# Rotary attention and a gated MLP: the first batch's loads and rotations moved between engines

## What is computed

```python
def rotate(x):
    x1, x2 = (x[..., :half], x[..., half:])
    return np.concatenate([x1 * cos - x2 * sin, x1 * sin + x2 * cos], axis=-1)
q_rot, k_rot = (rotate(q), rotate(k))
scores = scale * np.matmul(q_rot, k_rot.transpose(0, 1, 3, 2))
scores = scores - np.max(scores, axis=-1, keepdims=True)
attn = np.exp(scores)
attn = attn / (np.sum(attn, axis=-1, keepdims=True) + 1e-09)
x = np.matmul(attn, v)                    # heads side by side: (4, 576, 512)
h = np.maximum(x @ w_in, 0.0)             # (4, 576, 1024)
conv_out = sum over k of conv_w[k] * h shifted by k - 1 positions
y = (h * 1.0 / (1.0 + np.exp(-conv_out))) @ w_out
```

## Time and profile before

| | us |
|---|---|
| median of 3 runs | 656.71 |
| profiled execution | 655.78 |
| its span, first to last instruction | 653.7 |
| TensorE busy (matmul) | 515.2 (79%) |
| VectorE busy | 511.8 (78%) |
| ScalarE busy | 406.1 (62%) |
| GpSimd busy | 295.1 (45%) |
| mean granted TensorE clock | 0.957 of full |

### The profile page before, as it was taken

The page is one execution under the profiler, slowest core; times in us unless marked ns, Lnnn a source line. Parts: engine busy times, 40 slices in busy tenths (PEclk is TensorE's granted clock), DMA queues, the critical chain, the costliest instruction groups (busy, mean ns, idle before and its releaser), DMA issues.

```text
span 653.7 us, 11977 instructions
## 1 busy us (share of the span) xinstructions
PE 515.2 (79%) x3552; PEld 471.4 (72%) x3552; DVE 511.8 (78%) x882; ACT 406.1 (62%) x907; POOL 295.1 (45%) x329
## 2 busy tenths in 40 slices
PE   0068888889587888869687988888959888887987
PEld 0058776789586777769586867778958777777976
DVE  6978878579988888659997888848998788865652
ACT  1247988755556877745456787855555587875552
POOL 4414777734551456414451456523544145640221
PEclk9999999989799999999979999997979799999989
DMA  5976000314452000223454000041345200000011
GB/s 185 245 194 261 1 1 2 125 64 127 129 154 64 2 2 2 80 78 99 128 164 117 2 2 2 2 153 51 118 127 159 59 1 2 1 2 2 1 37 37
DMA packets 22773, 48.72 MB, mean 75 GB/s; under 512 B 3120, under 2 KB 7344, under 8 KB 21936
## 3 DMA queue, kind: packets, MB, share of 16 engines
q1 hardware_dynamic: 22704, 47.87, 24.1%
HBM read 28.98 MB, written 4.72 MB: 52 GB/s over the span
## 4 chain that ended last, share of the span: by engine, by line
PE 28%; DVE 28%; issue 18%; ACT 16%; DMA 5%; POOL 2%; SPq 1%; ACTq 1%; DVEq 0%; POOLq 0%
DVE conv L715 9%; PE banks L355 8%; DVE u L724 5%; PE banks L383 4%; ACT conv L553 3%; DVE PT_lo L702 3%; PE banks L386 3%; ACT P_first L499 3%; DVE Q L646 3%; PE banks L327 2%; ACT PT_hi L518 2%; PE banks L328 2%; ACT hid L545 2%; DVE neg_max L669 1%; DMA Q<-K 1%
## 5 line engine op out<-in xcount | busy, mean ns | idle before, releaser
L669 DVE TENSOR_REDUCE neg_max<-banks 128x1 f32<-128x576 f32 x144 | 108.5, 756 | 39.9 <-PE banks L328 34.1
L518 ACT ACTIVATE PT_hi<-banks 128x512 fp32r<-128x512 f32 (+1 forms) x160 | 95.1, 597 | 67.6 <-PE banks L355 63.3
L715 DVE SCALAR_TENSOR_TENSOR conv<-hid,taps,conv 128x288 f32<-128x288 f32 x128 | 97.3, 760 | 36.1 <-ACT conv L553 32.0
L327 PE MATMUL banks<-K,Q 128*128 128x288 f32 x256 | 86.3, 351 | 43.0 <-DMA K<-K 31.7
L867 POOL TENSOR_TENSOR u_lo<-u,u_hi 128x288 fp32r<-128x288 f32 x64 | 53.9, 844 | 133.2 <-ACT u_hi L564 133.2
L417 PE MATMUL banks<-u_hi,wo_hi 128*128 128x288 f32 x256 | 80.6, 315 | 40.8 <-ACT y_sb L570 25.6
L851 POOL TENSOR_SCALAR P_first<-P_first,recip 128x576 f32<-128x576 f32 x68 | 50.2, 747 | 126.5 <-DVE recip L686 126.5
L702 DVE TENSOR_TENSOR PT_lo<-banks,PT_hi 128x512 fp32r<-128x512 f32 x128 | 86.9, 684 | 25.0 <-ACT PT_hi L518 23.7
L355 PE MATMUL banks<-ident,P_first 128*128 128x128 f32 (+1 forms) x400 | 78.1, 292 | 27.6 <-DVE PT_lo L702 17.8
L383 PE MATMUL banks<-PT_hi,V 128*128 128x288 f32 x320 | 90.9, 314 | 1.4 <-DVE PT_hi L706 1.3
L327 PEld LDWEIGHTS banks<-K,Q 128*128 128x128 f32 x256 | 50.9, 199 | 52.6 <-issue 32.1
(11 more groups left out here) (75 smaller groups left out, 1304.0 us busy)
## 6 DMA issues: line engine op xcount, KB each, us to landing
xc<-qk_dram SPq DMA_DIRECT2D x28, 288.0 KB, 2.8
xs<-qk_swapped_dram SPq DMA_DIRECT2D x28, 288.0 KB, 3.8
v_raw<-v_rows_dram SPq DMA_DIRECT2D x4, 1280.0 KB, 5.4
KL<-Q SPq DMA_DIRECT2D x32, 144.0 KB, 3.6
Q<-K SPq DMA_DIRECT2D x32, 144.0 KB, 3.6
K<-K SPq DMA_DIRECT2D x32, 144.0 KB, 2.7
y_dram<-y_sb SPq DMA_DIRECT2D x8, 576.0 KB, 3.4
wi_raw<-w_in_dram SPq DMA_DIRECT2D x1, 2048.0 KB, 7.8
```

Source lines behind the costliest of these rows:

```text
L327: nc.tensor.matmul(out, Q[:, h, qc], K[:, h, cols], start=True, stop=False)
L518: nc.scalar.activation(PT_hi[0:m, kt, 0:FULL * 128], bank[0:m, :], ACT.Copy)\
L669: nc.vector.tensor_reduce(out=neg_max[:, c:c + 1], in_=banks[:, 2 * (t % 2):2 * (t % 2) + 2, 0:HALF], axis=AX.XY, op=ALU.max, negate=True) ...
L715: nc.vector.scalar_tensor_tensor(out=conv[:, n % 2, :], in0=hid[:, slot, first:first + HALF], scalar=taps[:, f, k:k + 1], in1=conv[:, n % ...
```

## The change

Only the first batch's preparation is touched:

- ScalarE issues the loads of all eight heads (`load_first`), SyncE the tables, the moves, and what comes behind them. SyncE's moves now go by pairs (`prepare_first`): both heads' KL, then both q, then both k.
- ScalarE loads the table of the exponential (`load_table`) ahead of its first high part.
- The product by sines is VectorE's (`rotate_first`), no longer GpSimd's.
- VectorE does heads 0 to 3 first, then the first two maxima; the rotations of heads 4 to 7 lie between the further first tiles (`first_maxima` with `between`). ScalarE's high parts and exponentials are ordered to fit.

```diff
+            def prepare_first():
+                for pair in range(PAIRS):
+                    two = (2 * pair, 2 * pair + 1)
+                    for j in two:
+                        sp.wait_ge(rope_lo, j + 1)
+                        move_kl(0, j)
+                    for j in two:
+                        move_q(0, j)
+                    for j in two:
+                        move_k(0, j)
+                    if pair == 0:
                         sp.dma_start(ident[:, :], ident_in).then_inc(consts_in, 16)
                         sp.dma_start(taps[:, :, :], conv_w).then_inc(consts_in, 16)
+                    if pair == 1:
                         sp.dma_start(v_raw[:, :, :, :], v_rows[0, :, :, :, :]).then_inc(v_in, 16)
...
-            prepare(0, starting=True)
+            prepare_first()
             load_weights(wi_raw, w_in, wi_in)
             load_weights(wo_raw, w_out, wo_in)
...
+            def load_first(j):
+
+                c, w = rope_buffers(j, True)
+                loaded = (qk_more_in if j % 4 >= 2 else qk_in)[j % 2]
+                if j >= 4:
+                    act.wait_ge(rope_lo, j - 3)
+                act.dma_start(c, qk[0, j, :, :]).then_inc(loaded, 16)
+                act.dma_start(w, qk_swapped[0, j, :, :]).then_inc(loaded, 16)
+
+            for j in range(4):
+                load_first(j)
             act.wait_ge(tables_in, N_TABLES)
-            for j in range(H):
-                rope_high(0, j, starting=True)
-            for tile in FIRST_TILES[:-1]:
-                exp_tile(0, *tile)
+            load_table(ACT.Exp)
...
             act.wait_ge(consts_in, N_CONSTS)
             act.wait_ge(rope_lo, H)
             attention(0, True)
...
-            def first_maxima(b):
+            def first_maxima(b, between=()):
+                rest = iter(between)
                 max_tile(b, 0, 0)
                 max_tile(b, 0, 1)
+                for j in itertools.islice(rest, 1):
+                    rope_first(j)
                 max_tile(b, 0, 2)
...
+            def rotate_first(j):
+                _, w = rope_buffers(j, True)
+                times_cos(0, j, starting=True)
+                nc.vector.tensor_tensor(w, w, sin_t[:, :], ALU.mult).then_inc(sin_done, 1)
+                rope_add(0, j, starting=True)
+
+            def rope_first(j):
+                rotate_first(j)
+                rope_low(0, j, starting=True)
...
-            first_maxima(0)
+            first_maxima(0, range(4, H))
...
             nc.gpsimd.memset(QT[:, :, :].bitcast(F32), 0.0).then_inc(zeroed, 1)
-            pool.wait_ge(tables_in, N_TABLES)
-            for j in range(H):
-                times_sin(0, j, starting=True)
```

More of the change, by code:

```diff
@@ L1 @@
+import itertools
 import concourse.bass as bass
@@ L230, in _, with load_qk @@
         def _(sp):
[L231 to L236, removed]
+            def load_qk(b, j):
+                c, w = rope_buffers(j, False)
+                sp.dma_start(c, qk[b, j, :, :]).then_inc(qk_in[j % 2], 16)
+                sp.dma_start(w, qk_swapped[b, j, :, :]).then_inc(qk_in[j % 2], 16)
             def move_kl(g, j):
@@ L257, in store_y, with prepare @@
                 sp.dma_start(y_out[b, :, :, half * HALF:(half + 1) * HALF], y_sb[:, :, :]).then_inc(y_stored, 16)
[L259 to L262, removed]
+            def prepare(b):
+                for j in range(2):
+                    load_qk(b, j)
                 for j in range(1, H + 3):
@@ L265, in prepare @@
                         sp.wait_ge(rope_lo, b * H + j)
[L266 to L271, removed]
+                        if j + 1 < H:
+                            load_qk(b, j + 1)
+                        move_kl(b, j - 1)
                     if 2 <= j <= H + 1:
@@ L275, in prepare @@
                         move_k(b, j - 3)
-                    if not starting and j == 6:
+                    if j == 6:
                         store_y(b - 1, 0)
-                    if starting and j == 5:
+            def prepare_first():
[9 more added lines that the diff above has]
+                    if pair == 0:
                         sp.dma_start(ident[:, :], ident_in).then_inc(consts_in, 16)
                         sp.dma_start(taps[:, :, :], conv_w).then_inc(consts_in, 16)
-                    if starting and j == 6:
+                    if pair == 1:
                         sp.dma_start(v_raw[:, :, :, :], v_rows[0, :, :, :, :]).then_inc(v_in, 16)
@@ L620, in weights_high @@
                 nc.scalar.activation(hi, raw, ACT.Copy).then_inc(w_hi_done, 1)
-            act.wait_ge(tables_in, N_TABLES)
-            for j in range(H):
-                rope_high(0, j, starting=True)
-            for tile in FIRST_TILES[:-1]:
-                exp_tile(0, *tile)
+            def load_first(j):
[7 more added lines that the diff above has]
+                load_first(j)
+            act.wait_ge(tables_in, N_TABLES)
+            load_table(ACT.Exp)
+            rope_high(0, 0, starting=True)
+            rope_high(0, 1, starting=True)
+            load_first(4)
+            load_first(5)
+            rope_high(0, 2, starting=True)
+            load_first(6)
+            rope_high(0, 3, starting=True)
+            load_first(7)
+            exp_tile(0, *FIRST_TILES[0])
+            exp_tile(0, *FIRST_TILES[1])
+            rope_high(0, 4, starting=True)
+            exp_tile(0, *FIRST_TILES[2])
+            exp_tile(0, *FIRST_TILES[3])
+            rope_high(0, 5, starting=True)
+            exp_tile(0, *FIRST_TILES[4])
+            rope_high(0, 6, starting=True)
+            rope_high(0, 7, starting=True)
             act.wait_ge(consts_in, N_CONSTS)
@@ L796, in first_maxima @@
                 reciprocals(b, 0, 2)
+                for j in rest:
+                    rope_first(j)
                 normalise_group(b, 2)
+            def rotate_first(j):
[6 more added lines that the diff above has]
+                rope_low(0, j, starting=True)
             def normalise_group(b, k):
```

16 lines of the change are left out of this document (8 added, 8 removed).

## The result

| | before | after |
|---|---|---|
| median of the comparison's runs, us | 656.75 (4 runs) | 669.79 (4 runs) |
| ratio | 1 | 1.0202, 95% interval 1.0156 to 1.0248 |
| profiled execution, span | 655.78, 653.7 | 670.29, 668.5 |
| mean granted TensorE clock | 0.957 | 0.937 |

The forecast was 660.5 (657.0 to 664.0). The sign was right, the time is outside the range. Neither of the two signs by which the prediction would have been wrong in kind came: the idle time ahead of the weights' copy is there, and what follows is later.

A forecast was written before the change was run, and what follows sets the result against it. It took VectorE's chain and the weights' landing as the late points, the later setting what follows: chain 0.2 later, weights +4.3 us. Added to 655.78 or 656.71, this gives 660.1 or 661.0; forecast 660.5 us, range 657.0 to 664.0.

The forecast's parts named there:

- two signs by which the prediction would have been wrong in kind: Idle time before the first weights' copy under 3 us, or present but later stages less than 3 us later.
- Start of VectorE: First product on head 0: put at 6.9 against 7.04, as the loads' own queue gains almost nothing.
- Rotations: All on VectorE: 3.75 us per head alone, heads 2 and 3 ending at 20.3, table load hidden.
- So I take 3.1 each.: Three chained moves on SyncE from 12.8, between 2.4 and 4.94 each: TensorE starts at 22.2 instead of 31.7.
- the meeting with GpSimd: GpSimd's four instructions on V, at about 34, slow VectorE's rotations by 0.9 us; head 7 ready at 46.9.
- Rival C: Loads hold the moves, 2.7 on top of 4.3: +7, 663.2 us; a half-clock stretch named at 0.8; chance 0.10.
- Weights: w_in's load waits behind head 7's moves: issued 52.3, landed 60.1 against 55.8, ScalarE waits 5.2 us; shift +4.3.
- The range: 8 in 10: 657.0 to 664.0 us, taking in most of rivals at 657.6 (chance 0.25) and 663.2 (0.10).
- the bound that had been worked out: First score on TensorE at 27.7 if each chained move takes 4.94 us, as one did behind loads.

The follow-up runs named there:

- e4: The kernel before, with SyncE issuing the weights' loads only when head 0's transposed tiles are all split: 669.67 us, ratio 1.0162.
- e2: The changed kernel, with ScalarE issuing the loads of heads 4 to 7 only after the moves of heads 0 and 1: 663.61 us, ratio 1.0090.
- e12: The changed kernel, with 11 float32 matmuls whose results nobody reads in TensorE's wait for the weights: 666.43 us, ratio 1.0101.
- e1: The changed kernel, with w_in's load issued right behind v's load, not behind the last moves: 660.45 us, ratio 1.0063.
- e6: The kernel before, with only the separate load queue, moves in pairs and early table load; sines stay on GpSimd: 661.65 us, ratio 1.0100.
- e3: The changed kernel, with w_in's load behind v's and the loads of heads 4 to 7 behind heads 0 and 1's moves: 657.26 us, ratio 1.0018.
- e8: The changed kernel, with all heads' loads issued at the start, w_in's load behind v's, and low parts not straight behind their sums: 656.73 us, ratio 0.9993.
- e11: The changed kernel, with 44 matmuls whose results nobody reads in TensorE's wait for the weights: 677.44 us, ratio 1.0306.
- e7: The kernel before, with only the first batch's products by sines moved to VectorE, in its old order: 655.20 us, ratio 0.9969.

## Why the prediction was wrong in size

- *Start of VectorE.* 7.49 instead of 6.9: the load of the small table of scales is now the one that lands last. 0.6 us, and 7.23 to 8.49 in the runs with this arrangement. Not all of it need be the change's: e4, with before's loads, started at 8.98.
- *Rotations.* Right: heads 2 and 3 ended at 21.4 (forecast 20.3, 0.6 of it the start), a rotation of heads 4 to 7 took 3.85 where nothing lay beside it (forecast 3.75), and the table load is hidden.
- ***"So I take 3.1 each."*** This step failed. The two queues did share the transfer engines, but the chain of three steps took 13.8 us from 12.73, not 9.3, and 8.1 in e2 without the loads. First score 26.55 against 22.2: **4.35 us**, which went through to head 7 (51.6 against 46.9, to 0.2) with 0.5 more for the meeting with GpSimd, 1.4 instead of 0.9. The Trainium skill, DMA: Bandwidth & Descriptors, section Queues, rings and completion order, says that an engine goes round its queues packet by packet. Q<-K at 3.62 against 4.94 on one common queue would fit, but in e12, whose transfers are the same, it took 4.68, so no run shows that the queue of its own made a move shorter. KL at 6.19, with 1.28 MB of loads beside it, shows that it is still far from free. Rival C had named this at 2.7.
- *Weights.* The rule was right to 0.1 in all: head 7 + 5.2 to the issue (forecast 5.4), + 7.9 to landing (7.8), 64.7. Before it stands 4.90 of waiting, forecast 5.2. Nothing gave it back (e1, e4). From 55.8 this makes 8.9, where 4.3 was forecast.
- *The clock.* The forecast had the stage behind the wait run as before. Rival C named a half-clock stretch behind the idle time at 0.8, but its +7 is 4.3 + 2.7 and leaves the 0.8 out. That price was near: the stretch behind the wait cost 1.4 us after, 1.2 in e4, and 0.7 in e2 and e6. What the prediction put at nothing is the second stretch, at 94 to 98 in dense work: 1.6 us after, in e3, e4 and e8 alike. It doesn't come of the wait alone: e2 and e6 wait 4.76 and 5.60 us and have none up to 130 us, e3 and e8 wait for no weights and have one. What brings it stays open. Rival C was thus the right case, with 4.35 and 3.0 against 2.7 and 0.8.
- *The range.* Its top, 664, left room for 3.5 of the 5.5 us between the value taken for the first score (22.2) and the bound that had been worked out (27.7). The bound itself held the measured 26.55. With that the forecast is 664.9 or so, and with the clock's 3.0 it is 668, near the 669.8.
- *Sum.* 8.9 by the weights and 5.6 by the rest make the profiled 14.5; the medians differ by 13.0. Of the rest, 3.0 are the two half-clock stretches. The last 2.5 are not settled; part of them is lost in the other kernels too (0.1 to 2.4).

## What to carry over

When a load stands on a queue behind a chain of small transfers, ask what the last link waits for: here one moved line (the weights ahead of the last moves) is worth 9 us in the slow order and some 0.3% in the old one. A queue of its own doesn't protect small chained moves from large loads; price them near the shared end, and put the loads where no chain runs, if the engine that needs them can spare the time (in e2 VectorE then waited 3.06 us). Where a wait empties TensorE, look at the granted clock behind it: one half-clock stretch cost 0.7 to 1.6 us here. Leave room in the range for such stretches elsewhere too.

## What the hardware showed that I had not expected

- A chain of three steps, each of two moves of 144 KB, 8.1 us alone, takes 13.8 beside loads on another queue, at 0.84 to 1.04 of the transfer engines. The first link suffers most: 6.19 us.
- TensorE's granted clock was 0.5 from 42 to 55 us when it had 20 matmuls to do there (after), and 1.00 in e11 with 18 and in e12 with 13, on nearly the same schedule, ahead of the filler. What decided it isn't shown.
- A half-clock stretch of TensorE well behind the sparse work (94 to 98 after) cost the same 1.6 us in four kernels (after, e3, e4, e8).
- Starting TensorE 8 to 11 us earlier bought nothing (e3, e8). In e3 VectorE's chain explains it (first low part 1.2 us later than before); in e8 the 1.2 us that head 1 had gained were lost by the end of the stretch at 102 to 106.
- VectorE's low part of 0.82 us took 1.43, and two normalised tiles 1.73 instead of 0.94, when GpSimd's instructions on v lay beside them (from 37.52 to 40.87). The Trainium skill, SBUF — State Buffer, section Who interferes with whom, says that a VectorE instruction with two inputs in SBUF contends with a GpSimd instruction that reads SBUF. e7, without GpSimd's products, has every product and sum of the rotations at 0.75 or 0.76, where before has 1.95 beside GpSimd, which agrees.
